# Row-sum reciprocals taken to all partitions through a scratch in DRAM, and a new order of work in the attention stage

## The reference

```
scores = q @ k.T / 8 + (cum_i - cum_j)      # cum = cumsum(log(clip(f)))
attn   = exp(scores - rowmax), causal
attn   = attn / (rowsum + 1e-9)
x      = attn @ v                           # 2304 tokens x 512
x      = relu(x @ w_in1)**2 @ w_out1        # 512 -> 2048 -> 512
out    = g(x @ w_in2) @ w_out2              # g: 0, (h+1)^2/4 or h
```

## Time and profile before

| | |
|---|---|
| profiled execution, time | 991.63 us |
| its span, first to last instruction | 989.8 us |
| TensorE busy, matmuls | 983.0 us (99%), 5266 matmuls |
| VectorE, ScalarE, GpSimd busy | 516.8, 405.3, 153.0 us |
| granted TensorE clock | 1.00 |
| DMA queue of SP | 49.37 MB, 15.6% of 16 engines' span |

### The profile page before, as it was taken

How to read it: one execution, slowest core, us unless ns; L and a number is a source line. 1 busy time by engine, 2 the same in 40 slices (tenths; PEclk the granted TensorE clock), 3 DMA queues, 4 the chain that set the end, 5 groups by cost and what they waited for, 6 DMA issues and landing times.

```text
span 989.8 us, 14986 instructions
## 1 busy us (share of the span) xinstructions
PE 983.0 (99%) x5266; PEld 859.0 (87%) x5266; DVE 516.8 (52%) x1079; ACT 405.3 (41%) x888; POOL 153.0 (15%) x208
## 2 busy tenths in 40 slices
PE   8999999999999999999999999999999999999998
PEld 7888888999988888888889998988888888888997
DVE  7888888765422332232233566555455445544544
ACT  7888888854322232232223454232222223223322
POOL 7877888600000000000000000000000000000000
PEclk9999999999999999999999999999999999999999
DMA  6445555232000000000002440000001000000100
GB/s 220 147 145 177 158 175 195 65 121 72 1 1 1 1 0 0 0 0 1 1 1 64 127 129 22 1 32 1 1 1 43 0 0 33 10 1 1 43 1 32
DMA packets 39473, 50.01 MB, mean 51 GB/s; under 512 B 2656, under 2 KB 26720, under 8 KB 39424
## 3 DMA queue, kind: packets, MB, share of 16 engines
q1 hardware_dynamic: 39424, 49.37, 15.6%
HBM read 44.56 MB, written 4.79 MB: 50 GB/s over the span
## 4 chain that ended last, share of the span: by engine, by line
PE 96%; DVE 2%; ACT 1%; issue 0%; DMA 0%
PE banks L1167 39%; PE banks L1198 19%; PE banks L1184 19%; PE banks L1121 7%; PE banks L1066 5%; PE banks L1076 5%; PE banks L1092 1%; PE banks L1125 1%; PE banks L1117 0%; ACT W L689 0%; DMA fs<-f_dram 0%; DVE W L894 0%; DVE r L928 0%; DVE r L922 0%; ACT r L716 0%
## 5 line engine op out<-in xcount | busy, mean ns | idle before, releaser
L1167 PE MATMUL banks<-xs,W 128*128 128x512 f32 (+1 forms) x1728 | 383.7, 371 | 0.0
L1167 PEld LDWEIGHTS banks<-xs,W 128*128 128x128 f32 x1728 | 317.9, 188 | 47.4
L1198 PE MATMUL banks<-W,gs 128*128 128x512 f32 x864 | 209.1, 390 | 0.2 <-DVE gs L905 0.2
L1184 PE MATMUL banks<-gs,W 128*128 128x512 f32 (+1 forms) x960 | 209.0, 367 | 0.0
L1184 PEld LDWEIGHTS banks<-gs,W 128*128 128x128 f32 x960 | 175.1, 188 | 22.5
L1198 PEld LDWEIGHTS banks<-W,gs 128*128 128x128 f32 x864 | 161.7, 188 | 32.9 <-DVE gs L905 0.5
L905 DVE TENSOR_TENSOR gs<-r,gs 128x512 fp32r<-128x512 f32 (+1 forms) x160 | 102.3, 639 | 113.0 <-ACT gs L710 62.1
L716 ACT ACTIVATE r<-r 128x512 f32<-128x512 f32 (+1 forms) x80 | 47.2, 590 | 217.2 <-DVE r L924 217.2
L912 DVE TENSOR_TENSOR r<-r 128x512 f32<-128x512 f32 (+1 forms) x80 | 51.0, 638 | 160.9 <-ACT r L707 160.9
L707 ACT ACTIVATE r<-banks 128x512 f32<-128x512 f32 (+1 forms) x80 | 44.3, 554 | 177.3 <-PE banks L1167 176.5
L922 DVE TENSOR_SCALAR r<-banks 128x512 f32<-128x512 f32 (+1 forms) x80 | 50.9, 636 | 76.0 <-PE banks L1167 75.7
(11 more groups left out here) (87 smaller groups left out, 692.7 us busy)
## 6 DMA issues: line engine op xcount, KB each, us to landing
qk_raw<-qk_dram SPq DMA_DIRECT2D x15, 608.0 KB, 6.2
W_raw<-moe_w_in_dram SPq DMA_DIRECT2D x32, 256.0 KB, 2.8
W_raw<-moe_w_out_dram SPq DMA_DIRECT2D x32, 256.0 KB, 3.0
cb<-cum_scratch SPq DMA_DIRECT2D x30, 256.0 KB, 4.4
v_raw<-v_dram SPq DMA_DIRECT2D x16, 320.0 KB, 5.3
cbt<-cum_scratch SPq DMA_DIRECT2D x30, 144.0 KB, 3.0
out_dram<-x SPq DMA_DIRECT2D x3, 1024.0 KB, 4.2
out_dram<-x SPq DMA_DIRECT2D x1, 768.0 KB, 3.5
```

What stands on the lines that cost most here:

```text
L1167: last = mm(h_ps(j, c, layer == 0), W[:, j, a, 0, t * P:(t + 1) * P], xs_of(layer, c)[:, b, t, 0:width(c)], start=(t == 0 and a == b), sto ...
L1184: last = mm(banks[:, t, 0:width(c)], W[:, j, a, 1, t * P:(t + 1) * P], gs[:, j % GR, b, 0:width(c)], start=(j == 0 and a == b == 0), stop= ...
L1198: last = mm(banks[:, t, :], gs[:, j % GR, a, t * P:(t + 1) * P], W[:, j, b, 1, :], start=(j == 0 and a == b == 0), stop=(j == FT - 1 and a ...
```

## The change

`rinv` is turned by one transpose into [9, 128], copied by one small ScalarE instruction to `rT`, stored by two DMAs of SP to a scratch in DRAM, and after these have landed read back by two DMAs that repeat each head's row over 64 partitions of `rbc`. The repeat into `rexp` and five of the six transposes go. The three orders are new, and so is the place of R in them: it now stands near the head of a step. In SP's queue the stores and loads for pair g - 3 stand between the load of `qk_raw` for pair g and the wait for the maxima.

```
-    NR = 2
...
+    PE_ORDER = [("T", 1, 1), ("T", 2, 1), ("S", 0, 0), ("S", 1, 0), ("R", 0, 1), ("O", 0, 1),
+                ("O", 1, 1), ("T", 3, 1), ("O", 2, 1), ("T", 4, 1), ("O", 3, 1), ("S", 2, 0),
+                ("O", 4, 1), ("T", 5, 1), ("O", 5, 1), ("T", 6, 1), ("S", 3, 0), ("S", 4, 0),
+                ("O", 6, 1), ("T", 0, 0), ("O", 7, 1), ("O", 8, 1), ("O", 9, 1)]
+    ACT_ORDER = [("S", 6, 1), ("S", 7, 1), ("S", 8, 1), ("T", 1, 1), ("T", 2, 1), ("R", 0, 1),
+                 ("T", 3, 1), ("S", 0, 0), ("T", 4, 1), ("S", 1, 0), ("T", 5, 1), ("S", 2, 0),
+                 ("T", 6, 1), ("S", 3, 0), ("S", 4, 0), ("T", 0, 0), ("S", 5, 0)]
+    DVE_ORDER = [("R", 0, 1), ("T", 1, 1), ("T", 2, 1), ("S", 0, 0), ("S", 1, 0), ("S", 2, 0),
+                 ("T", 3, 1), ("T", 4, 1), ("S", 3, 0), ("S", 4, 0), ("T", 5, 1), ("S", 5, 0),
+                 ("T", 6, 1), ("S", 6, 0), ("S", 7, 0), ("S", 8, 0), ("T", 0, 0), ("M", 0, 1),
+                 ("M", 1, 1)]
...
+    PE_LAST = [("T", 1, 1), ("T", 2, 1), ("U", 0, 1), ("O", 0, 1), ("O", 1, 1), ("T", 3, 1),
+               ("R", 0, 1), ("O", 2, 1), ("O", 3, 1), ("O", 4, 1), ("T", 4, 1), ("T", 5, 1),
+               ("O", 5, 1), ("U", 1, 1), ("U", 2, 1), ("T", 6, 1), ("O", 6, 1), ("U", 3, 1),
+               ("O", 7, 1), ("O", 8, 1), ("O", 9, 1)]
...
+            def spread_r(g):
+                sp.wait_ge(r_put, g + 1)
+                rows = sums[bass.ds(2 * g, 2), :]
+                sp.dma_start(rows[:, 0:QB * P].rearrange("h (i q) -> h i q", i=QB),
+                             rT[0:2 * QB, :]).then_inc(r_stored, 16)
+                sp.dma_start(rows[:, QB * P:S].unsqueeze(0),
+                             rT[2 * QB:2 * QB + 1, :].rearrange("a (h q) -> a h q", h=2)).then_inc(r_stored, 16)
+                sp.wait_ge(r_stored, 32 * g + 32)
+                for h in range(2):
+                    sp.dma_start(rbc[64 * h:64 * h + 64, :],
+                                 sums[bass.ds(2 * g + h, 1), :].broadcast_to([64, S])).then_inc(rbc_in, 16)
+
+            def reload(par, g, spread=None):
                 sp.wait_ge(qk_ready, g - 1)
                 load_qk(par, g)
+                if spread is not None:
+                    spread_r(spread)
                 sp.wait_ge(max_ready, NT * (g - 1))
                 load_cb(par, g)
                 sp.wait_ge(v_ready, g - 1)
                 load_v(par, g)
...
-            with sp.Fori(0, (PAIRS - 10) // 2) as m:
+            reload(0, 2)
+            reload(1, 3, 0)
+            with sp.Fori(1, (PAIRS - 10) // 2) as m:
                 for par in range(2):
-                    reload(par, 2 * m + 2 + par)
+                    reload(par, 2 * m + 2 + par, 2 * m + par - 1)
             for g in range(PAIRS - 8, PAIRS):
-                reload(g % 2, g)
+                reload(g % 2, g, g - 3)
...
             def put_r(par, g, n):
-                act.wait_ge(r_turned, NR * g + n + 1)
-                if n == 0:
-                    act.wait_ge(x_put, g + 1)
...
+                act.wait_ge(r_turned, g + 1)
+                act.wait_ge(x_put, g + 1)
+                nc.scalar.activation(rT[0:NT, :], banks[0:NT, ring_bank("R", n, par), 0:P], copy).then_inc(r_put, 1)
...
-                    dve.wait_ge(r_put, NR * (g + 1))
+                    dve.wait_ge(rbc_in, 16 * SPREADS * (g + 1))
...
+                pe.wait_ge(rinv_done, g + 1)
+                turn(ps[0:NT, 0:P], rinv[:, par, :], ident[:, :]).then_inc(r_turned, 1)
```

More of the change, by code:

```diff
@@ L37, in mixed_attention_mlp @@
     NT = len(TILES)
+    SUM_AT = [2 * QB if h == 2 else h * QB + i for h, i in TILES]
     PW = sum(WIDTH)
@@ new lines, in mixed_attention_mlp @@
+    PE_LAST = [("T", 1, 1), ("T", 2, 1), ("U", 0, 1), ("O", 0, 1), ("O", 1, 1), ("T", 3, 1),
[3 rows of a table added]
+    ACT_LAST = [("S", 6, 1), ("S", 7, 1), ("S", 8, 1), ("T", 1, 1), ("T", 2, 1), ("W", 4, 1),
+                ("T", 3, 1), ("R", 0, 1), ("T", 4, 1), ("W", 5, 1), ("T", 5, 1), ("G", 0, 1),
+                ("G", 1, 1), ("T", 6, 1), ("G", 2, 1), ("G", 3, 1)]
+    DVE_LAST = [("T", 1, 1), ("R", 0, 1), ("T", 2, 1), ("T", 3, 1), ("T", 4, 1), ("W", 4, 1),
+                ("W", 5, 1), ("T", 5, 1), ("G", 0, 1), ("G", 1, 1), ("T", 6, 1), ("G", 2, 1),
+                ("M", 0, 1), ("G", 3, 1), ("M", 1, 1)]
@@ L191, in mixed_attention_mlp @@
         rbc = at("rbc", [P, S], F32, 1)
-        rexp = at("rexp", [P, 2 * QB, DH], F32, 1)
+        rT = at("rT", [P, P], F32, 1)
         nmax = at("nmax", [P, 2, NT], F32, 1)
@@ L343, in mixed_attention_mlp @@
         rinv_done = sem("rinv_done")
-        rexp_done = sem("rexp_done")
         r_turned = sem("r_turned")
         r_put = sem("r_put")
+        r_stored = sem("r_stored")
+        rbc_in = sem("rbc_in")
         p_turned = sem("p_turned")
@@ L478, in reload @@
                 load_v(par, g)
-            with sp.Fori(0, (PAIRS - 10) // 2) as m:
+            reload(0, 2)
+            reload(1, 3, 0)
+            with sp.Fori(1, (PAIRS - 10) // 2) as m:
                 for par in range(2):
-                    reload(par, 2 * m + 2 + par)
+                    reload(par, 2 * m + 2 + par, 2 * m + par - 1)
             for g in range(PAIRS - 8, PAIRS):
-                reload(g % 2, g)
+                reload(g % 2, g, g - 3)
                 if g in (PAIRS - 8, PAIRS - 5, PAIRS - 3, PAIRS - 2):
                     load_w((PAIRS - 8, PAIRS - 5, PAIRS - 3, PAIRS - 2).index(g))
-            for n in range(FREE, 2 * FT):
+            spread_r(PAIRS - 3)
+            spread_r(PAIRS - 2)
+            early_w = (after_qk - FREE * SLOT) // SLOT
+            for n in range(FREE, FREE + early_w):
+                load_w(n)
+            spread_r(PAIRS - 1)
+            for n in range(FREE + early_w, 2 * FT):
                 load_w(n)
@@ L743, in do @@
                     put_r(par, g, n)
-                if what == "V":
-                    spread_r(par, g)
                 if what == "W":
@@ L1087, in turn_r @@
                 ps = banks[:, ring_bank("R", n, par), :]
[L1088 to L1092, removed]
-                                    rexp[:, u:u + 2, :].rearrange("p h d -> p (h d)"), ident[:, :])
-                else:
-                    pe.wait_ge(rinv_done, g + 1)
-                    turn(ps[:, 0:P], rinv[:, par, 0:1].broadcast_to([P, P]), ident[:, :])
-                    last = turn(ps[0:64, TAIL:TAIL + P], rinv[:, par, 0:1].broadcast_to([P, 64]), ident[:, :])
-                last.then_inc(r_turned, 1)
+                pe.wait_ge(rinv_done, g + 1)
+                turn(ps[0:NT, 0:P], rinv[:, par, :], ident[:, :]).then_inc(r_turned, 1)
             def product_v(par, g, n):
```

28 lines of the change are left out of this document (7 added, 21 removed), and 6 rows, old and new, of tables (PE_LAST, PE_ORDER).

## The result

The changed kernel takes 1010.21 us (median of 6, 1006.9 to 1014.46), the kernel before 991.83 us (median of 6). The ratio is 1.0186 with a 95% interval of 1.016 to 1.0211: 1.9% slower. I had said 997 and a range of 988 to 1003. The direction was right, the size was not: 18.4 us came where 5.5 were forecast. The profiled execution took 1007.71 us, 16.1 more than that of before, and its rows follow.

A forecast was written before the change was run, and what follows sets the result against it. TensorE's own issued work was taken to bound the kernel. Fourteen steps -0.3 us, weight tiles +5.8, first step +0.5 and last step -0.5 gave +5.5 on 991.63, so 997 us, range 988 to 1003.

The forecast's parts named there:

- TensorE's list: Sum of what TensorE issues in an attention step: 11.37 us after the change against 11.57, bounds 11.02 and 11.52.
- the third visit: In TensorE's step, scores on half of the rows come in three separate places, not two: 0.35 us more a step.
- the burst: Loads of decay, v and qk issued together each step, taken as 9.3 us, with the small stores served behind them.
- the inverse 0.55: VectorE's work on the row sums between M and T1's subtraction, taken as 0.55 us.
- The new path: From the landing of `rbc` through VectorE's M, inverse and T1 to TensorE's R in the next step: 2.55 us.
- The loop: Last maximum, DMA loads, stores, `rbc`, M, inverse, T1, R, next last maximum: 23.2 us over two steps, 11.55 taken a step.
- the weight tiles: 512 KB loads behind those for pairs 8, 11, 13, 14 delay `rbc`: 1.7 us each, 0.7 for one, 5.8 together.
- Start and last step: Pair 0's R needs all nine exponentials before O0, +0.5 us; the last step saves only transposes, -0.5 us.
- Worse: Rival: the store's way or the loads take 1 us more, 12.1 us a step, 1004 us; chance 0.12.
- The hidden case: Rival: `rbc` lands before the 11.4 us needed, also with weight loads; 989 us, or 984 without visit price; chance 0.25.

The follow-up runs named there:

- experiment 9: Changed kernel without the addition of 1e-9, the stores and loads of `rbc` ahead of the qk load, weight tiles behind the loads of `rbc`: 988.79 us, ratio 0.997.
- experiment 10: Kernel of experiment 9 with another TensorE order, visiting the half-row scores twice a step and not three times: 998.79 us, ratio 1.0069.
- Experiment 2: Changed kernel with the stores and loads of `rbc` ahead of the next qk load in SP's queue: 993.29 us, ratio 1.0017.
- 11: Changed kernel without the addition of 1e-9, and with the two small stores issued from ScalarE's DMA queue, not SP's: 997.12 us, ratio 1.0058.
- 5: Changed kernel without the addition of 1e-9, the reciprocal taken of the row sums directly: 997.63 us in a single run.
- 12: Kernel before the change, without the addition of 1e-9: 991.39 us, ratio 0.9996.
- 1: Changed kernel with the 1e-9 added by a tensor-tensor instruction from a constant tile, not a tensor-scalar one: 1009.14 us, ratio 1.0185.
- 14: Changed kernel without the addition, `rbc` stores and loads ahead of the qk load, weight tiles still in front of the stores: 989.98 us, ratio 0.9988.
- 4: Kernel before the change with the new orders of all engines, inverses spread on the chip, no trip through DRAM: 1012.83 us, ratio 1.0211.
- 13: Changed kernel with its addition, `rbc` stores and loads ahead of the qk load, weight tiles behind the loads of `rbc`: 991.62 us, ratio 1.0001.

## Why the prediction was right or wrong

**Right: what bounds, and the list as a sum.** I had 11.37 us for TensorE's list, from 0.55 less for five transposes and 0.35 more for the third visit. Undisturbed steps take 11.34 in the changed kernel and in experiment 9. The visit thus costs 11.34 - 11.57 + 0.55 = 0.32, if the transposes are worth what I took; no run shows the two apart, and experiment 10 speaks rather against it.

**Right: `rbc` comes behind the burst.** I had the stores served at the end of the burst, 5 us from issue to landing, and M waiting for the DMA in place of TensorE. The trace has 5.5 us in the step shown, 4.4 as a median, and M waits (L894) in 5 of the steps. Experiment 2 moves the qk load away and M's waits for `rbc` fall from 4.7 to 2.0 us, in 9 to 0.4. The reason that I borrowed from the Trainium skill, ring order within one queue, is not what delays the store: from another queue it is hardly sooner (11), 5.0 us as a median against 5.1 (5). The page itself has the sentence that fits, in "DMA: Bandwidth & Descriptors", section "Issuing engines are not separate DMA queues": DMAs of all issuing engines run on the same 16 DMA engines and interleave. The rows of experiment 11 agree.

**The step that failed: "the inverse 0.55".** In "The new path" I priced VectorE's way from the landing of `rbc` to TensorE's R at 2.55 us, with 0.55 for the inverse, read from one pair of rows, 0.37 for the addition and 0.22 for the reciprocal. The reciprocal is constant, the addition is not: 0.16 to 2.31 us, mean 0.92, 14.8 us in 16. The sum of before, 6.4, should have warned: the earlier trace rows has 0.37 where an undisturbed one takes 0.16. By the traces it ends with GpSimd's running instruction (72 of 72 that last longer than 0.2 us); GpSimd was busy for 22.05 of 25 us. In the old list it stood in the middle of the step, and taking it out there gained nothing (12). The new list puts it behind M, on the path to T1's bank, and M is late by the burst, so that the addition falls under GpSimd's subtraction of qk: in 10 of the 16 cases in the changed kernel, in none in experiment 2, where M is earlier. Leaving the addition out takes 12.6 us away (5).

The Trainium skill says this in "SBUF — State Buffer", section "Who interferes with whom": VectorE and GpSimd share a pair of SBUF ports as an exclusive lock held for the whole instruction, taken by VectorE in the two-port modes, which a tensor-scalar can enter, and for two SBUF inputs against a GpSimd instruction that reads SBUF; an instruction with one SBUF input outside these modes doesn't contend. The traces agree in all three: tensor-scalar up to 2.31 us, tensor-tensor from two SBUF tiles up to 2.36 (1), reciprocal 0.22 (5). That the port is the mechanism is argued from these ends and from the page; no run removed GpSimd's work, and no row shows an instruction's mode.

**Missing in the sum: the clock.** Nothing in it priced what a standstill of TensorE leads to. In the trace it stands still for 2.88 us at 129.34, and in the next step the granted clock is 0.50 for at least 6 us: this wait of 2.9 us costs some 3 us more. Those of 1.7 and 2.8 us cost 1.5 and 1.7 more; behind those of 1.1 the clock stays at 1.0. Over the span that is 7.0 us, and the executions scatter with it: 1006.9 us at a mean clock of 0.995, 1014.46 at 0.990. Where no TensorE wait is long (at most 0.8 in 2, none in 9), the clock is 1.0. The Trainium skill, "TensorE: Matmul & The Clock Gate", section "What's actually happening", names 1.2 GHz as the state of an idle engine and activity as what lifts it; the windows agree. The half clock and the waits were not varied apart, so the 7.0 are read from the clock column and not from a run of their own.

**The loop and the weight tiles.** I had the loop at 11.55 a step and 5.8 us for the weight tiles. With the addition out (5) the time is 997.6, near my 997, but that is in part luck. Of the 6.3 us of waits in its trace 2.5 are in usual steps, where the loop was to take 14 x (11.55 - 11.37) = 2.5, though in four single waits up to 1.4 and not 0.2 in each step. The other 3.8 are in three of the weight steps, where I had 5.8 for all; and the half clock behind the longest adds 1.7 that I had not counted. With qk moved, the weight tiles cost 1.2 (14 against 9). Start and last step I had at 0.5 and -0.5. In the changed kernel they and the 0.5 that lies in the steps with a wait are 16.1 + 3.2 - 11.5 - 7.0 = 0.8 together.

**The rivals.** "Worse" (1004, for a store or loads 1 us slower) was the nearest in size, but its cause was not the one found: the stores took 2.8 to 5.7 us, no more than the 5 or so of the forecast as a rule. The hidden case is what 9 makes of the kernel: 988.79, where I had 989. A loss of 12 us and more had 0.12 in my chances, and the mechanism that did it had nothing.

## What to carry to other kernels

A short VectorE instruction can be held up by GpSimd and then has no fixed duration: look at its shortest and longest beside its mean before it is moved to the head of a list that another engine waits for, and leave it where there is slack or use a form that isn't held up. Put small transfers on which compute waits ahead of big loads in time; another issuing queue did not help here (11). If TensorE will stand still for 2 to 3 us, count the half clock behind it as well (1.5 to 3 us each time here), and test two small losses together, for they can cost more than their sum.

## What the runs showed of the hardware that I had not expected

- An addition over nine columns, 0.16 us when nothing is in its way, lasted up to 2.31 us in the changed kernel and 2.69 in experiments 4 and 13, and ended within 0.04 us of GpSimd's instruction. The reciprocal in its place never did (0.203 to 0.218 us).
- The same 128 x 9 = 1152 reciprocals took 0.21 us as 128 partitions by 9 from SBUF and 0.94 as 9 by 128 from PSUM.
- From a store of 4 KB to the issue of its reader it took 5.1 us (median, up to 6.3) behind a burst, 5.0 (up to 6.7) from the other queue, and 2.7 (up to 3.5) without the last load in front (5, 11, 9).
- One standstill of 2.88 us was followed by at least 6 us at 1.2 GHz.
